# A linear-attention, MLP and expert kernel: who asks for the decay rates, and the order of work inside the attention tiles

## What is computed

```python
# q, k, v: (2, 8, 768, 64), lam: (8,)
intra = einsum('bhic,bhjc->bhij', qb, kb) * Dmask   # Dmask = lam ** (i - j) for i >= j
out   = einsum('bhij,bhjd->bhid', intra, vb) + einsum('bhid,bhde->bhie', qb * lam_pow, kv_state)
kv_state = lam_block * kv_state + einsum('bhsd,bhse->bhde', kb * rev_pow, vb)
...
x = moe(x)      # (silu(x @ w_gate) * (x @ w_val)) @ w_out, 512 -> 1536 -> 512
out = moe2(x)   # argmax router over 8 experts, relu(x @ w1[e]) @ w2[e], times the softmax gate
```

## Time and profile before

| | |
|---|---|
| median of 3 runs | 535.24 us (535.2 to 535.6) |
| the profiled execution | 536.05 us, of which the span is 534.3 us |
| PE busy in the span | 525.4 us (98%) |
| DVE, ACT, POOL busy | 353.3 (66%), 247.1 (46%), 74.4 us (14%) |
| PE's share of the chain that ended last | 95% |
| issue, DVE, POOL in that chain | 2%, 1%, 1% |

### The profile page before, as it was taken

How to read it: one execution, slowest core, us unless ns; L and a number is a source line. 1 busy time by engine, 2 the same in 40 slices (tenths; PEclk the granted TensorE clock), 3 DMA queues, 4 the chain that set the end, 5 groups by cost and what they waited for, 6 DMA issues and landing times.

```text
span 534.3 us, 8608 instructions
## 1 busy us (share of the span) xinstructions
PE 525.4 (98%) x3275; PEld 447.9 (84%) x3275; DVE 353.3 (66%) x609; ACT 247.1 (46%) x414; POOL 74.4 (14%) x94
## 2 busy tenths in 40 slices
PE   8999999999999999999999999999999999999995
PEld 7998888888888887887888888778999999999994
DVE  7889898796775647644556666567667666766620
ACT  4325464635354425442434544465555565555511
POOL 4991000000000000010000020023021130311001
PEclk9999999999999999999999999999999999999999
DMA  8997304213030305645244666267575656654001
GB/s 291 339 302 255 137 21 158 104 54 126 32 120 20 119 0 176 187 158 230 81 138 133 203 196 237 81 212 238 210 272 204 206 221 215 220 201 169 1 28 36
DMA packets 22281, 84.57 MB, mean 158 GB/s; under 512 B 3804, under 2 KB 3804, under 8 KB 18656
## 3 DMA queue, kind: packets, MB, share of 16 engines
q1 hardware_dynamic: 17376, 71.35, 39.0%
q0 software_dynamic: 3712, 10.54, 5.6%
q10 hardware_dynamic: 1152, 2.13, 1.0%
HBM read 75.59 MB, written 10.53 MB: 161 GB/s over the span
## 4 chain that ended last, share of the span: by engine, by line
PE 95%; issue 2%; DVE 1%; POOL 1%; POOLq 0%; ACT 0%
PE bank L934 18%; PE bank L859 16%; PE bank L1161 15%; PE bank L1171 12%; PE bank L867 12%; PE bank L891 6%; PE bank L1075 2%; PE bank L1094 2%; PE bank L783 2%; PE bank L821 1%; PE bank L794 1%; PE bank L1150 1%; PE bank L829 1%; PE bank L961 1%; PE bank L1204 1%
## 5 line engine op out<-in xcount | busy, mean ns | idle before, releaser
L1609 DVE TENSOR_TENSOR ewl<-stages,ewh 128x1024 fp32r<-128x1024 f32 x50 | 60.8, 1223 | 16.9 <-ACT ewh L1248 16.6
L1248 ACT ACTIVATE ewh<-stages 128x1024 fp32r<-128x1024 f32 x50 | 52.2, 1054 | 0.7 <-DMA stages<-expert_w 0.7
L1554 ACT ACTIVATE ehh<-bank 128x256 fp32r<-128x256 f32 x48 | 18.5, 385 | 58.1 <-PE bank L1161 58.0
L636 POOL DMA_DIRECT2D stages<-expert_w x8 | 4.6, 572 | 260.9 <-DVE more_hl L1609 185.3
L1171 PE MATMUL bank<-ewl,ehh 128*128 128x512 f32 x96 | 37.8, 394 | 0.0
L1171 PE MATMUL bank<-ewh,ehl 128*128 128x512 f32 x96 | 37.7, 393 | 0.0
L1171 PE MATMUL bank<-ewh,ehh 128*128 128x512 f32 x96 | 37.5, 391 | 0.0
L1161 PEld LDWEIGHTS bank<-exh,ewh 128*128 128x128 f32 x224 | 33.2, 188 | 3.6
L1161 PE MATMUL bank<-exh,ewh 128*128 128x256 f32 x224 | 36.0, 283 | 0.0
L2092 DVE SCALAR_TENSOR_TENSOR ehl<-bank,ehh 128x256 fp32r<-128x256 f32 x48 | 20.2, 422 | 23.8 <-ACT ehh L1554 23.7
L1161 PE MATMUL bank<-exl,ewh 128*128 128x256 f32 x224 | 34.9, 278 | 0.0
(11 more groups left out here) (291 smaller groups left out, 1248.6 us busy)
## 6 DMA issues: line engine op xcount, KB each, us to landing
stages<-expert_w SPq DMA_DIRECT2D x21, 1024.0 KB, 4.9
stages<-mlp_w SPq DMA_DIRECT2D x24, 768.0 KB, 4.5
stages<-attn_in SPq DMA_DIRECT2D x18, 512.0 KB, 5.6
stage<-expert_w SPq DMA_DIRECT2D x7, 1024.0 KB
stages<-expert_w POOLq DMA_DIRECT2D x8, 512.0 KB, 5.7
stage<-attn_in SPq DMA_DIRECT2D x6, 512.0 KB, 5.8
held<-c SPq DMA_DIRECT2D x12, 256.0 KB, 2.0
stages<-held SPq DMA_DIRECT2D x12, 256.0 KB, 2.8
```

Source lines behind the costliest of these rows:

```text
L1248: return nc.scalar.activation(dst, src, ACT.Copy)
L1554: nc.scalar.activation(ehh[f % 2][:, :], bank[:, H_BANK + f % 2, 0:CAP], ACT.Relu).then_inc(ehh_ready, 1)
L1609: V.tensor_tensor(dst, src, high.bitcast(F32), ALU.subtract).then_inc(inc, 1)
```

## The change

It does five things, all in the first 50 us of the program or, in the case of the router's weights, a load moved to a later place in SP's queue.

1. The transfer of the decay rates is issued by ACT, as the first thing it does, instead of by SP. SP begins with tile 0.
2. The router's weights are asked for after all attention tiles.
3. POOL does `queries(n)` before `keys(n)`.
4. `add_state(0)`, which closed DVE's pass n = 0, now stands behind the weighing of pass n = 1.
5. Of the four differences of tokens, which closed passes 8 to 11 of DVE's tile loop, the third now closes pass 11 together with the fourth.

```diff
--- before.py
+++ after.py
@@ -450,7 +450,6 @@
 
         @block.sync
         def _(sp):
-            sp.dma_start(lam_sb[:, :], lam_rows).then_inc(lam_landed, 16)
             def attention_in(s, n):
 
                 sp.dma_start(stage[s][:, 0:2 * DM], attn_in[n][:, 0:2 * DM]).then_inc(landed[s], 16)
@@ -458,11 +457,10 @@
 
             for s in range(4):
                 attention_in(s, s)
-                if s == 0:
-                    sp.dma_start(router[:, :, 0:E], router_w).then_inc(router_landed, 16)
             for n in range(4, NT):
                 sp.wait_ge(o_ready, n - 3)
                 attention_in(n % 4, n)
+            sp.dma_start(router[:, :, 0:E], router_w).then_inc(router_landed, 16)
 
             def load(key, f):
                 slot = LOAD_AT[key][0]
@@ -608,10 +606,10 @@
                                         ALU.mult).then_inc(faded_ready, 1)
 
             for n in range(1, NT):
+                if n >= 2:
+                    queries(n)
                 if n < LAST_STATE:
                     keys(n)
-                if n >= 2:
-                    queries(n)
                 if 2 <= n < LAST_STATE:
                     fade(n)
 
@@ -1304,6 +1302,7 @@
                 copy(xh[:, :, token_cols(n)],
                      bank[:, O_BANK[n % 2], :].rearrange("p (a i) -> p a i", a=NPAIR)).then_inc(xh_ready, 1)
 
+            act.dma_start(lam_sb[:, :], lam_rows).then_inc(lam_landed, 16)
             act.wait_ge(powers_step, 12)
             for a in range(NPAIR):
                 h = 2 * a + 1
@@ -1758,12 +1757,14 @@
                 weigh(n)
                 if n == NT - 1:
                     split_gate_val(0, 0)
+                if n == 1:
+                    add_state(0)
                 if n >= 1:
                     tokens_low(n - 1)
-                if n < LAST_STATE:
+                if 1 <= n < LAST_STATE:
                     add_state(n)
-                if n >= NT - 4:
-                    turn(1, n - (NT - 4))
+                for t in {NT - 4: (0,), NT - 3: (1,), NT - 1: (2, 3)}.get(n, ()):
+                    turn(1, t)
             split_out(0, 0)
             tokens_low(NT - 1)
             split_mlp(0, 1)
```

## The result

| | before | with the change |
|---|---|---|
| median | 535.47 us (6 runs, 535.2 to 536.3) | 539.04 us (6 runs, 538.78 to 540.09) |
| ratio, 95% interval | 1 | 1.0067 [1.0054, 1.0080] |
| the profiled execution, its span | 536.05, 534.3 | 539.11, 537.3 |

Predicted were 536.0, with a range of 533.8 to 536.6. A second measurement of both kernels gave 538.10 against 535.83 (1.0041 [1.0026, 1.0056]). The sign was right, and the size was +3.6 and +2.3 us instead of +0.8. The two spans differ by 3.0 us and the medians by 3.6, because the profiled execution of the kernel before lies 0.58 above its median and the other one 0.07.

The account below looks back on a forecast made before the run. PE was taken as the bound, busy throughout from 48.37 us, so the shift of the first MLP matmul counts. −0.2 − 0.5 − 0.65 + 2.13 = +0.78 us on the median 535.24 gave 536.0, range 533.8 to 536.6.

Parts of the forecast that it names:

- 0.47 us of lateness is free, and beyond it each microsecond costs one: At PE's to_state(0), waiting for ACT's kd: late lam costs 2.6 − 0.47 = +2.13 us.
- The size of the lateness: Lam's landing at the start: 2.6 us late, lower bound 0, upper 3.05.
- The reason for it: At the start's DMA: lam stands behind all of tile 0 on even one of 16 engines, landing with it at 5.13.
- Rival A: Lam's transfer gets through, waiting about 0.4 us for one packet, inside the free 0.47: sum −1.35, 533.9 us; chance 0.32.
- Tile 0 sooner: Start of scores(0): tile 0 issued at 0.83, landing at 5.1; −0.2 us, between 0 and −0.33.
- Queries ahead of keys: At tile 2: from_state(2) no longer waits for qs(2) behind kd(2) on POOL; −0.5 us.
- Second tile weighed, router last: DVE's tile 1 and SP's loads: 0 each; router up to +0.3 us if the MLP weights land later.
- The end: Last tiles: one xt leaves ahead of tile 11's pt, and the first xt may shorten (0.2 more); −0.65 us, −0.4 to −0.8.
- rival C: Lam late and end gain eaten by router pieces delaying MLP weights and moved xt delaying first product: 536.7 us; chance 0.10.

Follow-up runs that it names:

- combined: Kernel before plus lam issued by ACT with SP held for POOL's first signal, queries ahead of keys, add_state(0) behind tile 1's weighing: 535.21 us, 0.9990.
- sp_held: Changed kernel, but SP waits for POOL's first memset before asking for tile 0, so lam on ACT goes first: 535.84 us, 1.0001.
- queries_only: Kernel before with only POOL's queries(n) put ahead of keys(n): 535.54 us, 0.9994.
- lam_act_only: Kernel before with only lam's transfer moved from SP to ACT: 538.51 us, 1.0052.
- rest_lam_sp: Changed kernel with lam's transfer back at the head of SP's queue: 535.80 us, 1.0003.
- turns_back: rest_lam_sp with the differences of tokens back where they stood in the kernel before: 535.50 us, 0.9997.
- after_warm: Changed kernel with keep_busy(15) instead of keep_busy(3) ahead of to_state(0), filling PE's wait with matmuls: 537.66 us, 1.0039.

## Why the prediction was wrong

**The step that failed** is the price of lam's lateness: "0.47 us of lateness is free, and beyond it each microsecond costs one". In the profile after, each microsecond cost one up to `to_state(0)`, and then PE worked at 1.2 GHz for about 3 us and paid about 1.4 us more, for which the sum had no term. The forecast named the idle time itself ("PE waits about 2 us") and the two durations of the same matmul, 0.24 and 0.145 us, and didn't put them together. The Trainium skill (TensorE: Matmul & The Clock Gate, Part 1: The HAM clock gate) says that an idle PE falls back to its lower clock; the rows agree, with waits of 2.90 and 2.52 us followed by 0.50, and one of 1.80 that wasn't.

**The size of the lateness** was 2.6 in the sum with 3.05 as its bound. Five traces of the tie, with lam on ACT, gave 3.16, 2.55, 2.68, 2.79 and 2.55. In the trace that was timed first it was the worst, 0.56 of the miss.

**The reason for it was half right.** That lam lands with tile 0 held. That it stands behind the whole of tile 0 on an engine did not: the two queues alternate, 83 packets to 84, as the Trainium skill (DMA: Bandwidth & Descriptors, Issuing engines are not separate DMA queues) has it of transfers from SP and ACT. The earlier trace rows were misread: from 268.6 to 268.9 us, where both queues have packets, they were served alike there too, 18 and 19 of them. Why ACT's first one came 2.8 us after its issue stays open; it was a store of 260 KB.

```profile
q1 hardware_dynamic: 18, 0.05, 44.4%
q10 hardware_dynamic: 19, 0.04, 33.6%
```

Rival A had the rule and mispriced it, by letting lam wait for one packet. It is nine packets on each engine, and it waits for one of tile 0 with each.

**Tile 0 sooner**, −0.2: it landed at 5.5 and not at 5.1 (4.7 us from the issue, where it took 4.3 before). PE's row ahead of `to_state(0)` ended at 10.18 instead of 10.59, and PE waited there for `kd`. With `kd` on time `to_state(0)` starts 0.53 earlier in `combined` and 0.02 earlier in `sp_held`, although tile 0 is asked for at the same time in both. The moment at which the clock rises at the start moves between executions: the 16 matmuls of `scores(0)` take between 1.16 and 2.06 us in these profiles. So one profile can't size this term.

**Queries ahead of keys**, −0.5: 0.53 in `queries_only`, and `from_state(2)` follows `within(1)` by 0.93 in the changed kernel as forecast (17.52 to 18.45). But beside a late lam it is no gain of its own. `lam_act_only` has the queries behind the keys, and takes the same 3.97 us from `to_state(0)` to `from_state(2)`: there POOL finds tile 2 landed, does the `kd` of both tiles in a row from 12.34 and ends `qs` at 15.65, well before PE comes at 16.56. In the kernel before POOL had waited 1.78 us for that tile. So the wait would have gone in the changed kernel without this part too.

**Second tile weighed, router last**, 0: nothing seen of either; the first was never run alone.

**The end**, −0.65: −0.90 in the changed kernel, but mostly not by the mechanism that was priced. The `xt` of pass 8 took 0.69 us, not 1.75, because POOL's `qs`, from 40.37 for 1.18, had ended when it began (the smaller part of the forecast's term); in `combined` the two overlap again and it takes 2.15. From `from_state(11)` to the first MLP matmul it is 2.59 us in the kernel before, `queries_only` and `combined`, with a long `xt`. It is 2.04 in `lam_act_only`, where that `xt` is short (0.72) and no difference has moved, and 1.85 in the changed kernel. So by these two the moved difference has at most 0.19 of it. In the pair that tests it alone it gave 0, but there `gvl` starts as ACT's `gvh` ends (46.45 after 46.42, 45.94 after 45.90), so the weights' transfer hides what it may give. It cost 0.25 at the second unit, which the forecast had named and priced only in rival C.

So the sum read −0.2 + 2.13 for the start, where +2.56 was measured; −0.5 for the wait at tile 2, which went; 0 for the clock, where +1.4 was measured; −0.65 for the end, −0.90; and 0 behind it, +0.25 and 0.2 more that no landmark explains.

## What to carry to other kernels

A small transfer on which everything hangs needs a head start on the shared engines, not a queue of its own: here, 0.22 us ahead it lands in 1.7 us, and in a tie with 512 KB it takes 4.3 to 4.9 from ACT's queue and 3.1 from SP's. When a forecast makes PE wait for microseconds, price the matmuls behind the wait at the lower clock too, and think of filler work on PE if the wait must stay. Work moved off one late engine's queue lands on its next deadline: count the room there before it is booked as a gain. And a gain of half a microsecond at the start reaches the end only if the next transfer on the way also comes sooner: follow the chain that ended last in the new trace.

## What was not expected of the hardware

- Two queues with work at the same moment were served one packet for one packet in sum, whatever the size: 83 of 4 KB and 84 small ones in 1.2 us. A 6 KB transfer in 144 packets took as long as its 512 KB neighbour, 4.9 us against 4.7.
- How a tie begins depends on the side: by 2.7 us, 3 packets of lam had passed with lam on ACT, 109 with lam on SP, issued 0.01 us ahead.
- After PE idled for 2.5 to 2.9 us the granted clock read 0.50 for more than 3 us; after 1.8 us it did not fall in the one profile there is. Over the whole span it was 0.994 to 0.996 in all six executions of the changed kernel's first measurement, where a stretch of 3.4 us at half takes 0.003 away (an estimate, 3.4 × 0.5 / 537), and 0.995, 0.996, 0.996 and 0.998 in its second; the kernel before has 0.997 to 1.000. So it seems to fall in nearly all of them; the execution at 0.998, 537.89 us, is only 0.1 to 0.4 shorter than the other three, so a single one can't be sorted by this figure.
- A `xt` on DVE takes 0.69 us alone. In eight traces it is held up by a POOL instruction beside it, and in each of them it ends 0.54 to 0.56 us after that one's end: 1.75 us long in the kernel before, 1.51 in `rest_lam_sp`. The 2.15 in `combined` are two of POOL's: the `xt` starts at 37.14 while `faded` runs (36.56 for 1.04), `qs` follows at 37.56 and ends at 38.73, the `xt` at 39.29. In `turns_back` and `after_warm` it is the other way round: the `xt` keeps its 0.69, and the `qs` beside it takes 1.68 instead of 1.18. The Trainium skill (SBUF — State Buffer, SBUF: two separate sides) says that such a pair takes turns at a shared port for whole instructions; these rows agree. Which of the two gets in first can't be told from start times that lie 0.02 to 0.07 us apart.
